# Three attention blocks and a seven-product matrix scheme on one core: filler matmuls in the first block made 512 columns wide, four products moved into it, keys stored once

## The reference

```python
# attention: batch 4, heads 8, 768 rows, head width 64; 32-row chunks
for c in range(nc):
    k_ctx = k[:, :, max(0, 32*c - 16):min(S, 32*c + 40)]
    k_full = np.concatenate([mem_k, k_ctx], axis=2)      # 8 memory keys
    scores = scale * np.matmul(q_c, k_full.transpose(0, 1, 3, 2))
    ...                                                  # row softmax
    out[:, :, c_start:c_end] = np.matmul(a, v_full)
x = ...                                                  # [3072, 512]
gate = 1.0 / (1.0 + np.exp(-(x @ w_gate)))               # 512 x 1536
x = gate * (x @ w_val) @ w_out                           # 1536 x 512
# second stage: h = x @ w_in (512 x 2048), g = P(h) / Q(h), out = g @ w_out
```

## Time and profile before

| what | value |
| --- | --- |
| time, median of 3 runs | 1188.41 us (1186.41 to 1194.03) |
| time of the profiled execution | 1185.17 us |
| span of the profiled execution | 1183.2 us |
| granted TensorE clock, mean | 1.000 |
| busy PE, DVE, ACT, POOL | 98%, 78%, 64%, 11% |

### The profile page before, as it was taken

The page is one execution under the profiler, slowest core; times in us unless marked ns, Lnnn a source line. Parts: engine busy times, 40 slices in busy tenths (PEclk is TensorE's granted clock), DMA queues, the critical chain, the costliest instruction groups (busy, mean ns, idle before and its releaser), DMA issues.

```text
span 1183.2 us, 20934 instructions
## 1 busy us (share of the span) xinstructions
PE 1162.0 (98%) x8076; PEld 956.3 (81%) x8076; DVE 926.8 (78%) x1419; ACT 751.8 (64%) x1224; POOL 125.4 (11%) x150
## 2 busy tenths in 40 slices
PE   9999999999999998999999999999999999999998
PEld 8878888777888777788887888888888888888887
DVE  5875676777567677766657898998988988988987
ACT  2565555456555544655556787877877877877865
POOL 2123222012322201133200000000000000000000
PEclk9999999999999999999999999999999999999999
DMA  8522322842232283332219200200200200200000
GB/s 286 155 56 78 143 80 65 283 121 94 77 142 81 63 279 116 127 105 72 80 40 324 73 1 1 72 1 1 71 0 0 71 0 0 71 0 0 36 1 36
DMA packets 40721, 97.60 MB, mean 82 GB/s; under 512 B 4288, under 2 KB 4288, under 8 KB 40640
## 3 DMA queue, kind: packets, MB, share of 16 engines
q1 hardware_dynamic: 40640, 96.49, 24.6%
HBM read 83.89 MB, written 12.58 MB: 82 GB/s over the span
## 4 chain that ended last, share of the span: by engine, by line
PE 57%; DVE 1%; DMA 1%; SPq 0%; issue 0%; ACT 0%; ACTq 0%
PE ps_h L1294 7%; PE ps_h L1293 7%; PE ps_h L1298 7%; PE ps_y L1333 7%; PE ps_y L1337 7%; PE ps_y L1331 7%; PE ps_h L1186 3%; PE ps_h L1188 3%; PE ps_h L1193 3%; PE ps_y L1231 1%; PE ps_y L1236 1%; PE ps_y L1232 1%; DMA oraw<-wo_l 1%; PE ps_y L1326 0%; PE ps_y L1327 0%; PE ps_y L1325 0%
## 5 line engine op out<-in xcount | busy, mean ns | idle before, releaser
L1186 PE MATMUL ps_h<-xop,wop 128*128 128x512 f32 x504 | 197.3, 391 | 4.9 <-DVE x_raw L829 2.3
L1188 PE MATMUL ps_h<-xop,wop 128*128 128x512 f32 x504 | 196.2, 389 | 0.0
L1193 PE MATMUL ps_h<-xop,wop 128*128 128x512 f32 x504 | 155.6, 390 | 0.0
L1293 PE MATMUL ps_h<-x_split,weights 128*128 128x512 f32 x384 | 149.4, 389 | 0.0
L1294 PE MATMUL ps_h<-x_split,weights 128*128 128x512 f32 x384 | 149.4, 389 | 0.0
L1331 PE MATMUL ps_y<-weights,hid 128*128 128x512 f32 x360 | 140.0, 389 | 0.0
L1333 PE MATMUL ps_y<-weights,hid 128*128 128x512 f32 x360 | 140.0, 389 | 0.0
L1186 PEld LDWEIGHTS ps_h<-xop,wop 128*128 128x128 f32 x504 | 94.6, 188 | 28.2 <-DVE x_raw L829 4.0
L829 DVE TENSOR_TENSOR x_raw<-ps_h,probs_t 128x512 f32<-128x512 f32 x72 | 49.3, 685 | 85.9 <-PE ps_h L1193 85.9
L687 ACT ACTIVATE tmp<-ps_h 128x512 f32<-128x512 f32 x96 | 57.2, 596 | 92.4 <-PE ps_h L1298 92.4
L808 DVE TENSOR_TENSOR wop<-rawp,wop 128x448 fp32r<-128x448 f32 x144 | 85.7, 625 | 33.9 <-ACT wop L443 33.9
(11 more groups left out here) (92 smaller groups left out, 2278.9 us busy)
## 6 DMA issues: line engine op xcount, KB each, us to landing
rawp<-wgv_l SPq DMA_DIRECT2D x36, 512.0 KB, 3.7
oraw<-wo_l SPq DMA_DIRECT2D x72, 256.0 KB, 3.9
unit<-k_l SPq DMA_DIRECT2D x24, 512.0 KB, 5.5
unit<-v_l SPq DMA_DIRECT2D x24, 512.0 KB, 4.8
unit<-q_l SPq DMA_DIRECT2D x24, 256.0 KB, 4.2
x_stage<-y_dram SPq DMA_DIRECT2D x6, 1024.0 KB, 5.9
out<-stage SPq DMA_DIRECT2D x24, 256.0 KB, 2.2
braw<-wb_l SPq DMA_DIRECT2D x11, 512.0 KB, 5.9
```

What stands on the lines that cost most here:

```text
L1186: nc.tensor.matmul(dst, w_h[k], xop[:, m, 0, k, :], start=first and k == 0, stop=False, skip_group_check=True)
L1188: nc.tensor.matmul(dst, w_l[k], xop[:, m, 0, k, :], start=False, stop=False, skip_group_check=True)
L1193: last = nc.tensor.matmul(dst, w_h[k], xop[:, m, 1, k, :], start=False, stop=k == 1, skip_group_check=True)
L1293: nc.tensor.matmul(dst, lhs(c, 0), x_split[:, 0, c, :], start=(c == 0), stop=False)
```

## The change

Five things are edited. (1) `warm_up` multiplies 128x512 zeros of the 32-bit matmul type instead of the identity; there are twelve before the first unit and three at most places, and they wait for a `memset` on POOL. (2) M1 and M2 of chains 0 and 1 run inside attention 0 (`early_product`), in banks of `ps_y`; the splits that they need come earlier on ACT and DVE. (3) The keys of a tile are stored once, with the 8 memory keys after each chunk: 184 columns for a head instead of four windows of 64, so a load of keys is 368 KB instead of 512 KB; `scores` reads overlapping windows. (4) At each change of block ACT takes the snapshot of M1 earlier, DVE splits the outer weights after the two chain sums, and POOL makes the weight sums of chains 2, 14 and 26 only after all token splits. (5) In attentions 1 and 2 one third of pair 0 moves from behind `weigh_values` of the first unit to ahead of its `turn`.

```diff
-                nc.tensor.matmul(ps_y[:, 0, 256:256 + P], ident[:], ident[:], start=True, stop=True)
+                nc.tensor.matmul(ps_y[:, 3, :], warm[:, 0:P], warm, start=True, stop=True)
...
+            def early_product(c, m):
+                pe.wait_ge(w_lo, 4 * c + m + 1)
+                product(c, m)
...
-                for m, (w, name, first) in enumerate(STEPS):
+                for m in range(M6 if c < 2 else M1, PROD):
...
+            def fill_first(p, place):
+
+                if (p, place) == (3, 4):
+                    early_product(0, M1)
+                    early_product(0, M2)
+                elif (p, place) == (4, 0):
+                    early_product(1, M1)
+                elif (p, place) == (4, 1):
+                    warm_up(WARM)
+                    early_product(1, M2)
+                elif place != 2:
+                    warm_up(2 * WARM if (p, place) == (0, 1) else WARM)
+
+            pe.wait_ge(warm_done, 1)
+            warm_up(4 * WARM)
             pe.wait_ge(ident_done, 2)
-            warm_up(2 * WARM)
-            attention(0, lambda: warm_up(WARM))
+            attention(0, fill_first)
...
-                def fill():
-                    third(*divmod(next(thirds), 3))
+                def fill(p, place):
+                    if p == UNITS // 2:
+                        few = 1 if place == 0 else 4
+                    else:
+                        few = 1 if (p == 0 and place in (2, 4)) or (p, place) == (3, 4) else 2
+                    for _ in range(few):
+                        third(*divmod(next(thirds), 3))
```

The banks of chains 0 and 1:

```diff
-        def bank_of(kind, name):
-            return {"P": 0 if kind == 0 else 3, "Q": 1, "R": 2}[name]
+        def bank_of(c, name):
+
+
+            if c < 2 and name != "R":
+                return ps_y[:, 2 * c + "PQ".index(name), :]
+            return ps_h[:, {"P": 0 if c % 2 == 0 else 3, "Q": 1, "R": 2}[name], :]
```

On POOL, ACT and DVE:

```diff
+                if c % CHAINS == 2:
+                    pool.wait_ge(xa_lo, XOPS * (c // CHAINS + 1))
...
             def last_operands(s, between):
                 between(0)
+                if s == 0:
+                    snapshot(0, 0)
                 split_x(s, T3, 0)
                 split_x(s, T4, 0)
                 split_x(s, T2, 1)
+                if s:
+                    snapshot(CHAINS * s, 0)
                 split_x(s, T1, 1)
+                split_x(s, B22, 1)
                 between(1)
-                split_x(s, B22, 1)
                 between(2)
...
                     split_x(s, T4, 1)
-                    split_wout(n + 2)
                 else:
...
                 chain_sum(cg, 1)
                 chain_sum(cg, 2)
+                if i == 0:
+                    split_wout(n + 2)
```

And in `at_start` the token operand B11 is split at (p, place) = (2, 1) on ACT and (2, 2) on DVE, B21 at (2, 2) and (3, 0), each a place or two earlier than before; the keys' loads and windows:

```diff
-        k_raw = [unit[:, s, NQC:NQC + NKC] for s in range(2)]
+        k_raw = [unit[:, s, NQC:NQC + HP * NKEYS] for s in range(2)]
...
+                        window = slice(STEP * chunk_at[c], STEP * chunk_at[c] + KEYS)
...
-                                k_sb[b][D * e:D * (e + 1), c, h, :], start=True, stop=True)
+                                k_sb[b][D * e:D * (e + 1), h, window], start=True, stop=True)
```

More of the change, by code:

```diff
@@ L440, in split_w @@
                     act.wait_ge(raw_loaded[c % 2], 16 * (c // 2 + 1))
[L441 removed]
+                    if c > 1:
+                        act.wait_ge(m_done, products(c - 2, M4))
                 act.wait_ge(s_made, 4 * c + (0, 1, 3, 4)[i])
@@ L1153, in warm_up, with product @@
                 for _ in range(products):
-                    nc.tensor.matmul(ps_y[:, 0, 256:256 + P], ident[:], ident[:], start=True, stop=True)
+                    nc.tensor.matmul(ps_y[:, 3, :], warm[:, 0:P], warm, start=True, stop=True)
+            def product(c, m):
+                s, (w, name, first) = c // CHAINS, STEPS[m]
+                dst = bank_of(c, name)
+                w_h, w_l = [[wop[:, c % 2, part, 256 * w + P * k:256 * w + P * (k + 1)] for k in range(2)]
+                            for part in range(2)]
+                if c % CHAINS == 0:
+                    pe.wait_ge(xa_hi, XOPS * s + HI_NEED[m])
+                for k in range(2):
+                    nc.tensor.matmul(dst, w_h[k], xop[:, m, 0, k, :], start=first and k == 0, stop=False,
+                                     skip_group_check=True)
+                    nc.tensor.matmul(dst, w_l[k], xop[:, m, 0, k, :], start=False, stop=False,
+                                     skip_group_check=True)
+                if c % CHAINS == 0:
+                    pe.wait_ge(xa_lo, XOPS * s + LO_NEED[m])
+                for k in range(2):
+                    last = nc.tensor.matmul(dst, w_h[k], xop[:, m, 1, k, :], start=False, stop=k == 1,
+                                            skip_group_check=True)
+                last.then_inc(m_done, 1)
+            def early_product(c, m):
+                pe.wait_ge(w_lo, 4 * c + m + 1)
+                product(c, m)
             def chain(c, n):
```

157 lines of the change are left out of this document (78 added, 79 removed).

## The result

| | before | after |
|---|---|---|
| median of 5 runs each, same chip, us | 1188.41 (1186.41 to 1194.03) | 1179.8 (1179.45 to 1184.26) |
| ratio | | 0.9948 [0.9923, 0.9973] |
| profiled execution, us | 1185.17 | 1184.26 |
| its span, us | 1183.2 | 1182.2 |

The changed kernel is 0.5% faster, 6.2 us by the ratio and 8.6 by the medians. On a second chip it stood at 0.9936 [0.9914, 0.9958]. The forecast was a time of 1174.5 and a gain of 12.6 us from the profiled execution: the time is inside the range, the gain is half to two thirds of what the sum gave. The profiled execution took the longest of the five of its kernel, so it can't be set beside the one of before as a whole; it is read stage by stage.

What follows compares the result with a forecast made beforehand. TensorE, busy or filling 98% of the span, was taken as the bound. Gains 5.9 + 2.2 + 4.5 = 12.6 us gave 1172.6 from the profiled execution, 1175.8 from the median; forecast 1174.5 between them, range 1169 to 1182.

Steps and rivals of the forecast that it cites:

- Attention 0, gain 5.9: Attention 0: less filling ends the last staging at 49.0 us instead of 54.90, gain 5.9 us (3.9 to 7.9).
- Three are 0.68 us in place of 1.5: Filling in attention 0: three wide products at 0.228 us each replace 1.5 us, so a TensorE unit takes 3.7 us.
- the loop's 4.17: Attention 0: the dependency loop through all engines takes 8.3 us for two units, 4.17 for one, and becomes the bound.
- The sum from the first row maximum to the end of the last staging, 40.7 us: Attention 0: this stretch takes 40.7 us against 48.6 before, with 1.1 us of halts added separately.
- The steps of 4.17, 4.45, 5.25, 6.65 and 7.7: Attention 0: 4.17 us for each of four steps, then units 4, 5 and 6, then last row maximum to staging.
- They sat on the bound; now half of them find slack: Attention 0: of some 2.2 us of TensorE halts without a releaser, 1.1 us (0 to 2.2) still costs time.
- The rival that attention 0 stays near its pace: Attention 0: units stay near 5.3 us, only 2 of 5.9 us gained, about 1178.5 us; chance 0.12.
- That the clock falls in attention 0: Rival: dense filling drops TensorE to 1.2 GHz in attention 0, slower than before, 1188 to 1194 us; chance 0.05.
- Smaller key loads at nothing: Key loads of 368 instead of 512 KB: no gain, since loads are asked for two units, 8.3 us, ahead.
- Chains 0 and 1, gain 2.2: Chains 0 and 1: M4 of chain 0 earlier by 0.9 us, 1.3 more at chain 1; 2.2 us (1.0 to 3.5).
- Changes of block, gain 1.7 + 2.4: Second and third change of block: M6 stops waiting, token splits escape POOL's sums; 1.7 and 2.4 us.
- Moved third, 0.4: Attentions 1 and 2: the third fills a 0.8 us wait, which moves to ScalarE's copy, leaving 0.2 us each.

Runs made afterwards that it cites:

- the four with narrow filling: Filling by 128x128 identity products: kernel before (1188.41 us), it with changes of block (1181.84), changed kernel so filled (1182.39), that with early products behind attention 0 (1181.07).
- lighter loads: Changed kernel with loads of units 2 to 7 cut to 64 KB: values only (1179.45 us), or queries, keys and values each (1176.86 us).
- the kernel with the blocks alone: Kernel before plus only the later POOL weight sums, earlier snapshot and `split_wout` behind the chain sums: 1181.84 us, ratio 0.9959.
- the kernel shifted by 18: Changed kernel with 9 small products (18 matmul records) added where TensorE waits ahead of the first `turn`: 1179.31 us, ratio 0.9928.
- the kernel with four products: Changed kernel with four wide filling products at a place of attention 0 instead of three: 1180.71 us, ratio 0.9955.
- the kernel shifted by 64: Changed kernel with ten wide and 33 small products at the start instead of twelve wide, moving later matmuls 64 records: 1186.16 us, ratio 0.9994.
- the kernel with the hidden shift of 36: Changed kernel with 18 small products (36 matmul records) added where TensorE waits ahead of the first `turn`: 1179.43 us, ratio 0.9933.

## Why the prediction was right or wrong

**Attention 0, gain 5.9: failed.** By the medians the rework of TensorE's program gives nothing that can be measured, between 1.9 us gained and 2.0 lost, chains included, and wide filling alone loses 2.6. The start was forecast well: the twelve wide products took 5.31 us, `scores` started at 6.56 (6.3 forecast) and the first row maximum at 7.45 (7.2). The steps behind it:
- "Three are 0.68 us in place of 1.5": mis-sized. 0.228 us is the distance within a row of products of one kind; a group of three between others takes 0.91 to 0.98. A unit on TensorE is 4.39 us, not 3.7, and so TensorE stays the bound, ahead of VectorE's 4.13 and of the loop's 4.17. Cost: some 0.2 us a unit from the second step on; the first took 4.14.
- The sum from the first row maximum to the end of the last staging, 40.7 us without halts: right where loads are light (49.78 + 0.60 - 7.07 = 43.3 us, of it 2.7 halts, leaves 40.6). The steps of 4.17, 4.45, 5.25, 6.65 and 7.7 were there, halts and all, 4.14 to 5.22, 5.06, 5.53, 6.63 and 7.80. Unit 6, the seventh, does wait for ScalarE's staging behind the splits, as forecast, by up to 1.33 us.
- "They sat on the bound; now half of them find slack", with 0 to 2.2 us of halts: this is the step that failed. With the full loads and wide filling they are 0.9 to 6.4 us, 3.4 and more in eleven of thirteen profiles (2.2 to 3.9 in the four with narrow filling). TensorE waits there for instructions. An estimate from the rows above: a packet starts 2.5 us after a boundary on average, takes 1.0, and TensorE goes on some 1.4 after its landing, 4.9 us in all for 127 records. At 4.39 us for a unit of 138 records TensorE is there after 4.0 us; in the kernel before, with 156 records in 5.31 us, after 4.3. A faster TensorE comes to the boundary sooner, and the packet doesn't.
- Behind a long halt comes the clock, which the sum left at full speed. Over the whole of all profiles fourteen halts are of 1.8 us and more, and behind twelve of them the granted clock went to 0.50, 1.2 GHz, for 3.4 us or more. Two of the twelve are in attention 1 of kernels with narrow filling (2.62 and 2.18 us). In all thirteen profiles with full loads and wide filling attention 0 or chains 0 and 1 had such a stretch, and one of the four with narrow filling had one. I had priced halts as a fixed sum taken over from before, and the clock as a rival of its own that dense filling would bring on. The runs show them tied together: the clock mostly fell behind a long idle time, and a long halt is one.

The rival that attention 0 stays near its pace, "since the halts without a releaser and loads follow TensorE's speed", 0.12 and 1178.5 us, is what happened, within 1.3 us of the time. That the clock falls in attention 0 was in the list with 0.05, with dense filling as the reason, and it came in stretches, not throughout. The two profiles with wide filling and lighter loads, whose halts are all under 1.1 us, had none, which speaks for the idle times and against the filling by itself.

**Smaller key loads at nothing: failed.** They are worth some 4.7 us in the changed kernel, by one pair of medians on one chip. "Loads are asked for two units ahead" covers the wait for data, and that wait was indeed small. It doesn't cover what the loads do to others: with less traffic the last staging came 2 to 5 us earlier in two of two profiles of the changed kernel, and 2.1 in the one of the kernel before.

**Chains 0 and 1, gain 2.2: right in mechanism, smaller.** From the last staging to the first output third 25.8 us instead of 27.1: 1.3 gained, of which the kernel with the blocks alone, where `split_wout` stands behind the sums too, has 0.9. M4 of chain 0 came 11.1 us after the staging's end (10.8 forecast), the new wait at M6 of chain 1 is 1.27 us (1.35), but the wait at M4 of chain 1 grew from 0.76 to 1.18. That M1 and M2 no longer standing behind the attention "is not their gain" holds only beside the order of before; in the changed order putting them back costs 2.9 us.

**Changes of block, gain 1.7 + 2.4: right.** 5.0 us by the medians, interval 2.8 to 7.0, of which some 0.9 belongs to chains 0 and 1. No wait came up at M5, M7 or M3 there.

**Moved third, 0.4: right in mechanism, its size not measurable.** Its wait went to ScalarE's copy, 0.82 us at 208.95, and with the third put back the time is the same within what can be told apart.

**The sum** was 12.6 us with 5.9 on attention 0. By kernels of which each adds one part to the last, it was 4.9 for the blocks (ratio 0.9959), a loss of 2.0 with the rework and the moved third (0.9976), and 4.7 for the smaller key loads (0.9936), together 7.6 us. With an interval of 2 to 3 us each way for each step, only the blocks and the key loads are clear of nothing. The time came into the range since a term of 5.9 that failed was made up in part by one of 4.7 that I had put at nothing: that is luck.

## What to carry to other kernels

Filling between small matmuls is not spare time that can be cut: cutting it brings TensorE sooner to instructions that have not come, and behind such a long wait the work mostly ran at half the clock. In one profile each, two waits of 1.2 us were cheaper than one of 2.3. Price a shortened stage by a run in which the traffic beside it is taken away, and by the rows of the same group in the same company, not by the best distance within a long row. And bytes that nobody waits for can still cost: with a DMA share of 0.74, as in the first 37 us here, the instructions themselves come in beside them. A halt with no releaser can be checked: look for a packet on the instruction queue that lands 1.2 to 1.6 us ahead of its end.

## What was not expected of the hardware

- TensorE halts at every 128th matmul of its program at most, at places that a shift of the program moves exactly, for 0 to 2.6 us, and goes on 1.2 to 1.6 us after a packet of 16384 bytes has landed on the instruction queue. With a DMA share of 0.20 from 20 to 55 us, instead of 0.53 to 0.65 in the seventeen profiles with the full loads, no halt in attention 0 was over 1.1 us. Why a packet starts late beside loads is not shown.
- The granted clock fell to 0.50 behind idle times of 1.81, 1.90, 1.91 and 2.28 us, and stayed there for 3.4 to 6.8 us even though TensorE worked almost without a gap. It isn't a rule of length alone: it stayed at 1.00 behind a halt of 2.43 us in the kernel shifted by 18, behind one of 2.00 in the kernel with four products (218.25 us), and behind a wait of 2.43 for VectorE in the kernel before with wide filling (50.91 us). And it fell behind one of 1.63 in the kernel shifted by 64 (22 to 30 us, 0.57), and for 10.2 us from 37.2 on in the kernel with the hidden shift of 36, where two waits of 1.33 us and one of 1.18 had come within 10 us.
- Matmuls of 64 rows by 32 columns that write the same place took 0.055 us for each record at the start; the same form in `scores`, with changing places, takes 0.012, and 0.018 in the slow rows at 5.13 us of the kernel before. How much of the rest is the same place was not tested.
